# Top-k attention and two MLPs on one core: scores in native float32 by row halves, and other token pieces

## The reference

```python
# q, k, v: (4, 8, 576, 64); top_k = 32
scores = scale * np.matmul(q, k.transpose(0, 1, 3, 2))
kth = np.partition(scores, -top_k, axis=-1)[..., -top_k:-top_k + 1]
scores = np.where(scores >= kth, scores, -1000000000.0)
attn = np.exp(scores - np.max(scores, axis=-1, keepdims=True))
attn = attn / (np.sum(attn, axis=-1, keepdims=True) + 1e-09)
x = np.matmul(attn, v)                        # then (2304 tokens, 512)
gate = 1.0 / (1.0 + np.exp(-(x @ w_gate)))    # 512 -> 1536
y = gate * (x @ w_val) @ w_out                # -> 512
r = np.maximum(y @ w2_in, 0.0)                # -> 2048
out = (r * r) @ w2_out                        # -> 512
```

## Time and profile before

| | us |
|---|---|
| median of three runs | 1310.2 (1307.43 to 1312.79) |
| profiled execution | 1313.2 |
| its span | 1311.4 |

### The profile page before, as it was taken

How to read it: one execution, slowest core, us unless ns; L and a number is a source line. 1 busy time by engine, 2 the same in 40 slices (tenths; PEclk the granted TensorE clock), 3 DMA queues, 4 the chain that set the end, 5 groups by cost and what they waited for, 6 DMA issues and landing times.

```text
span 1311.4 us, 22472 instructions
## 1 busy us (share of the span) xinstructions
PE 1208.8 (92%) x7744; PEld 1083.6 (83%) x7744; DVE 842.9 (64%) x1692; ACT 807.9 (62%) x1806; POOL 654.1 (50%) x619
## 2 busy tenths in 40 slices
PE   3669888878998979999999999999999999999999
PEld 2558777878998879999989888887788888887999
DVE  6886796846767765787899567677863444640121
ACT  5986766757677766765786677657764443541221
POOL 6974557655655845552674455435634431430221
PEclk9779898989999989999999999999999999999999
DMA  5894665666666476655566554554455645556998
GB/s 187 315 311 132 213 223 197 217 237 230 233 228 212 169 261 240 216 191 190 176 215 214 205 181 155 187 181 157 155 182 200 208 167 174 172 174 197 344 364 302
DMA packets 89249, 279.08 MB, mean 213 GB/s; under 512 B 9904, under 2 KB 11952, under 8 KB 89136
## 3 DMA queue, kind: packets, MB, share of 16 engines
q1 hardware_dynamic: 89136, 277.65, 61.5%
HBM read 237.24 MB, written 40.37 MB: 212 GB/s over the span
## 4 chain that ended last, share of the span: by engine, by line
PE 69%; DMA 9%; POOL 8%; ACT 7%; issue 4%; DVE 2%; SPq 1%; ACTq 0%; POOLq 0%; DVEq 0%
PE ps L486 18%; PE ps L488 17%; PE ps L487 17%; PE ps L421 4%; PE ps L405 4%; PE ps L393 4%; DMA raw<-qk_in 4%; DMA ring<-w_in 3%; PE ps L472 3%; DMA w_split<-ring 2%; POOL ring L735 2%; POOL below L740 2%; POOL klo L721 1%; POOL qkh L726 1%; PE ps L415 1%
## 5 line engine op out<-in xcount | busy, mean ns | idle before, releaser
L740 POOL TENSOR_TENSOR below<-scores,below 128x576 f32<-128x576 f32 x144 | 207.3, 1440 | 247.1 <-ACT below L538 246.8
L659 DVE MAX8 top<-work 128x8 f32<-128x576 f32 x432 | 313.1, 753 | 4.9
L486 PE MATMUL ps<-xy_hi,ring 128*128 128x512 f32 (+3 forms) x800 | 290.0, 362 | 2.5 <-POOL xy_lo L764 1.7
L488 PE MATMUL ps<-xy_hi,ring 128*128 128x512 f32 (+3 forms) x800 | 282.9, 354 | 0.0
L487 PE MATMUL ps<-xy_lo,ring 128*128 128x512 f32 (+3 forms) x800 | 282.7, 353 | 0.0
L661 DVE MATCH_REPLACE8 work<-top,work 128x576 f32<-128x576 f32 x288 | 214.0, 743 | 0.0
L486 PE MATMUL ps<-g_hi,ring 128*128 128x512 f32 (+3 forms) x560 | 202.7, 362 | 2.9 <-POOL ring L735 2.8
L488 PE MATMUL ps<-g_hi,ring 128*128 128x512 f32 (+3 forms) x560 | 197.9, 353 | 0.0
L487 PE MATMUL ps<-g_lo,ring 128*128 128x512 f32 (+3 forms) x560 | 197.9, 353 | 0.0
L486 PEld LDWEIGHTS ps<-xy_hi,ring 128*128 128x128 f32 x800 | 151.0, 189 | 22.0 <-issue 6.2
L686 DVE SCALAR_TENSOR_TENSOR full_buf<-act_buf,ps 128x512 f32<-128x512 f32 (+3 forms) x60 | 35.6, 594 | 206.8 <-PE ps L488 201.8
(11 more groups left out here) (67 smaller groups left out, 2212.0 us busy)
## 6 DMA issues: line engine op xcount, KB each, us to landing
ring<-w_split SPq DMA_DIRECT2D x318, 512.0 KB, 3.8
w_split<-ring SPq DMA_DIRECT2D x68, 512.0 KB, 3.8
ring<-w_in SPq DMA_DIRECT2D x113, 256.0 KB, 3.5
vt<-v_in SPq DMA_DIRECT2D x32, 320.0 KB, 3.4
raw<-qk_in SPq DMA_DIRECT2D x16, 480.0 KB, 4.7
raw<-qk_in SPq DMA_DIRECT2D x16, 448.0 KB, 4.3
raw<-qk_in SPq DMA_DIRECT2D x8, 576.0 KB, 6.2
raw<-qk_in SPq DMA_DIRECT2D x8, 512.0 KB, 4.5
```

The lines of the kernel that those rows point to most:

```text
L486: nc.tensor.matmul(dst, w_hi, hi[:, k, 0:WIDTH[c]], start=first, stop=False)
L488: mm = nc.tensor.matmul(dst, w_lo, hi[:, k, 0:WIDTH[c]], start=False, stop=final)
L659: nc.vector.max(out=best, in_=sc if step == 0 else wk).then_inc(sel_step[t % 2], 1)
L740: nc.gpsimd.tensor_tensor(out=below[:, t % 2, :], in0=scores[:, t % 4, :], in1=below[:, t % 2, :], op=ALU.subtract).then_inc(mask_done, 1)
```

## The change

- The pieces become 128, 256, 384, 512, 512 and 512 tokens. There are still 144 tiles and 80 units with 16 halves; the MLPs start at slots 11, 28, 52, 84 and 116, and the last piece's 512 tokens come after attention. There are 36 groups instead of 32.
- Scores are native float32 matmuls straight from the loaded data. `heads_in` holds q twice (rows 0 to 63 and 64 to 127), the first half of the keys on rows 0 to 63 and the second on rows 64 to 127. A tile is two matmuls of 64 rows and 288 columns, one for each half of the rows, into different banks; a half tile is four, of 64 rows by 64 stationary columns.
- `split_head` goes from ScalarE and GpSimd, and so do `raw`, `qkh` and `klo`. A group's two heads are loaded two groups ahead, after the scores of the group that used the buffer.
- RING goes from 6 to 8 and AHEAD from 4 to 5; the first 23 splits begin at slot 0 instead of 2. GpSimd's `split_x` comes after the first evacuations of a slot.
- `pe_ns`, by which `shares()` deals out the MLP, is as before.

```diff
-CHUNK_BLOCKS = (3, 6, 7, 8, 8, 4)
+CHUNK_BLOCKS = (2, 4, 6, 8, 8, 8)
...
-RING = 6
-AHEAD = 4
+RING = 8
+AHEAD = 5
...
-for _g in range(1, NG):
-    for _h in range(2):
-        HEADS_AT.setdefault(max(FIRST_TILE[_g] - 5 + _h, FIRST_TILE[_g - 1] - 2, 0), []).append((_g, _h))
+for _g in range(2, NG):
+    HEADS_AT.setdefault(max(FIRST_TILE[_g - 1] - 2, 0), []).append(_g)
...
-    SPLIT_AT.setdefault(2 + _k // 2, []).append(_k)
+    SPLIT_AT.setdefault(_k // 2, []).append(_k)
...
+            def load_heads(g):
+                if g >= 2:
+                    sp.wait_ge(s_scored, FIRST_TILE[g - 1])
+                for h in range(2):
+                    sp.dma_start(heads_in[:, 2 * (g % 2) + h, 0:B64 * GROUPS[g][4] + HALF],
+                                 qk_of(g, h)).then_inc(heads_loaded[g % 2], 16)
...
             def score(t):
                 u, part = TILES[t]
                 g, i = UNITS[u][1], UNITS[u][3]
-                heads = [0, 1] if part == 2 else [part]
-                pe.wait_ge(qk_lo_done, 2 * g + heads[-1] + 1)
+                pe.wait_ge(heads_loaded[g % 2], 32 * (g // 2 + 1))
                 wait(pe, s_copied, t)
-                q = q_columns(g)
-                for half in range(2):
-                    dst = ps[:, half, 0:HALF]
-                    done, steps = 0, 2 * len(heads)
-                    for h in heads:
+                q = B64 * GROUPS[g][4]
+                for step in range(2 if part == 2 else 1):
+                    for half in range(2):
+                        rows = slice(DH * half, DH * half + DH)
+                        if part == 2:
+                            h = (half + step) % 2
+                            out_rows, n = slice(B64 * h, B64 * h + B64), B64
+                        else:
+                            h, out_rows, n = part, slice(0, P), P
                         r = 2 * (g % 2) + h
-                        at = P * i + (B64 if part == 2 and h == 0 else 0)
-                        for rhs in (qkh[:, r, q + half * HALF:q + (half + 1) * HALF],
-                                    klo[:, r, half * HALF:(half + 1) * HALF]):
-                            mm = nc.tensor.matmul(dst, qkh[:, r, at:at + P], rhs, start=(done == 0),
-                                                  stop=(done == steps - 1))
-                            done += 1
+                        mm = nc.tensor.matmul(ps[out_rows, half, 0:HALF], heads_in[rows, r, P * i:P * i + n],
+                                              heads_in[rows, r, q:q + HALF], start=True, stop=True)
                 mm.then_inc(s_scored, 1)
...
-                for g, h in HEADS_AT.get(s, []):
-                    split_head(g, h)
```

More of the change, by code:

```diff
@@ L58 @@
 CHUNK_END = [max(END[u] for u in range(NU) if UNITS[u][0] == c) for c in range(NC)]
[L61 to L70, removed]
+QMAX = max(B64 * GROUPS[g][4] for g in range(NG))
+QK_AT = [sum(2 * P * (B64 * GROUPS[h][4] + HALF) for h in range(g)) for g in range(NG + 1)]
 VCOLS = 2 * KFULL * DH + P
-QK_AT = [sum(2 * P * (q_columns(h) + SEQ) for h in range(g)) for g in range(NG + 1)]
 KT = 4
@@ L183, in sem @@
             return ctx.enter_context(nc.semaphore(name))
-        raw = sb("raw", [P, 2, QMAX + SEQ])
-        qkh = sb("qkh", [P, 4, QMAX + SEQ], F32R)
-        klo = sb("klo", [P, 4, SEQ], F32R)
+        heads_in = sb("heads_in", [P, 4, QMAX + HALF])
         vt = sb("vt", [P, 2, VCOLS])
@@ L232, in qk_of @@
         def qk_of(g, h):
-            cols = q_columns(g) + SEQ
+            cols = B64 * GROUPS[g][4] + HALF
             at = QK_AT[g] + h * P * cols
@@ L248, in attention_mlps @@
         const_ready = sem("const_ready")
-        raw_loaded = [sem("raw_loaded0"), sem("raw_loaded1")]
+        heads_loaded = [sem("heads_loaded0"), sem("heads_loaded1")]
         v_loaded = [sem("v_loaded0"), sem("v_loaded1")]
@@ L255, in attention_mlps @@
         w_lo_done = sem("w_lo_done")
-        qk_hi_done = sem("qk_hi_done")
-        k_lo_done = sem("k_lo_done")
-        qk_lo_done = sem("qk_lo_done")
         s_scored = sem("s_scored")
@@ L348, in mlp_dma @@
                                      act_buf[:, m % 2, 0:WIDTH[c]]).then_inc(out_stored[m % 2], 16)
-            load_head(0, 0)
-            load_head(0, 1)
+            load_heads(0)
+            load_heads(1)
             load_v(0)
@@ L358, in _ @@
                     mlp_dma(blocks_of(SHARES[s - 1][2]))
-                for g, h in (HEADS_AT.get(0, []) if s == 0 else []) + HEADS_AT.get(s + 1, []):
-                    load_head(g, h)
+                for g in HEADS_AT.get(s, []):
+                    load_heads(g)
                 if s in V_AT:
@@ L513, in _ @@
         def _(act):
[L514 to L521, removed]
             def copy_scores(t):
@@ L618, in _ @@
             nc.scalar.activation(rp[:, 0, 0:1], ident[:, 0:1], ACT.Exp)
-            split_head(0, 0)
-            split_head(0, 1)
             copy_scores(0)
@@ L716, in _ @@
         def _(pool):
[L717 to L729, removed]
             def split_weights(k):
@@ L803, in _ @@
                     normalise(UNIT_AT[s - NORM])
+                for c, n in blocks_of(SHARES[s - 1][2]) if s else []:
+                    evac(c, n)
                 for c, p in X_AT.get(s, []):
                     split_x(c, p)
[L806 to L809, removed]
                 for k in SPLIT_AT.get(s, []):
@@ L826 @@
     kt = k.reshape(heads, SEQ, DH).transpose(0, 2, 1)
-    qk_a = np.zeros(QK_AT[NG], np.float32)
+    qk_a = np.empty(QK_AT[NG], np.float32)
     for g, (c, b, p, at, n, col) in enumerate(GROUPS):
-        fc, qc = full_columns(g), q_columns(g)
-        part = qk_a[QK_AT[g]:QK_AT[g + 1]].reshape(2, 2, DH, qc + SEQ)
+        qc = B64 * n
+        part = qk_a[QK_AT[g]:QK_AT[g + 1]].reshape(2, 2, DH, qc + HALF)
         for h in range(2):
             hd = b * HEADS + 2 * p + h
-            part[h, :, :, :fc] = qt[hd, :, B64 * at:B64 * at + fc]
-            if n % 2:
-                part[h, :, :, fc + B64:fc + 2 * B64] = qt[hd, :, B64 * at + fc:B64 * (at + n)]
-            part[h, :, :, qc:] = np.roll(kt[hd], B64 * h, axis=1)
+            part[h, :, :, :qc] = qt[hd, :, B64 * at:B64 * at + qc]
+            part[h, :, :, qc:] = np.roll(kt[hd], B64 * h, axis=1).reshape(DH, 2, HALF).transpose(1, 0, 2)
     v_in = v.reshape(heads // 2, 2, SEQ, DH)
```

## The result

The changed kernel takes 1360.95 us (median of 4 runs, 1360.26 to 1364.21) where the kernel before takes 1311.49: the ratio is 1.038, with a 95% interval of 1.034 to 1.042. The forecast was 1288, with a range that ended at 1335. The profiled execution has a span of 1358.3 us.

A forecast was written before the change was run, and what follows sets the result against it. Bounds: the attention chain to 102.1 us, late split weights to 503.4, then TensorE. Start 71, small stages 302, then 212 + 264 + 250 + 190 made 1289 us of span, time 1288, range 1248 to 1335.

The forecast's parts named there:

- What bounds the kernel now: Whole kernel before: attention chain to 102.1 us, late split weights to 503.4, then TensorE, busy for all but 8.2 us.
- The start: Attention before the first MLP matmul: 71 us for 102.1, VectorE's 5.5 us a tile being late next.
- Two row halves at once: Full score tile: its two native matmuls on different rows overlap, 0.48 us of work instead of 0.97.
- The rival that they do not overlap: Score tiles: halves run one after the other, 0.48 us more a tile, 1342 us in all; chance 0.12.
- its milder form: Score tiles: halves overlap only in part, 0.24 us more a tile, 1315 us; no chance of its own.
- The switch of tiling: Score tiles: entering and leaving row tiling costs about 0.1 us each way, 0.19 a tile, 0.67 with the work.
- Half tiles: The 16 half tiles: 1.15 us each with quarters run in pairs (0.67 if four at once), for 1.06 before.
- SyncE's queue in the 128-token stage: Every third block costs 3.8 us of landing and 4 x 0.43 of issue; with 12 other DMAs 132 us.
- Rival B: Small stages: SyncE's queue and stores bind more; landings 1.5 us later add 36 us, 1325 in all; chance 0.16.
- The factor of 1.2 on TensorE's need: 128- and 256-token stages: TensorE's need of 252 us times the earlier stages' 1.2 gives 302, bounds 265 and 340.
- Ring of 8, splits 5 ahead: 256-token stage: loads asked for two block steps earlier, so ScalarE's 38.6 us of waiting falls under 10.
- The sum: Whole kernel: the stretches' forecasts add up to 1289 us of span for 1311.4, time 1288.

The follow-up runs named there:

- e1: The kernel before with only the new pieces and first splits from slot 0 (old scores, ring of 6, splits 4 ahead): span 1402 us, ratio 1.067.
- e4: The changed kernel with ring of 6 instead of 8 and splits 4 ahead instead of 5: span 1384 us, ratio 1.058.
- e7: The changed kernel with both key halves multiplied from rows 0 to 63: stretches 3 to 5 took 228.1, 288.0, 264.7 us for 213.0, 273.0, 252.5.
- e9: e5 with splits 3 blocks ahead instead of 5: median 1300.36 us, ratio 0.993 to the kernel before.
- e5: The changed kernel with the refill behind a store issued three block steps after it instead of one: span 1312 us, ratio 1.005 to the kernel before.
- e6: e5 with the old pieces 192, 384, 448, 512, 512, 256: median 1274.87 us, ratio 0.972 to the kernel before.

## Why the prediction was wrong, step by step

- *What bounds the kernel now:* right. TensorE after 503 us, the making of split weights in the small stages.
- *The start:* forecast 71, measured 64.3. The term "0.1 to 0.2 us a slot" for the splits of q and k was the wrong size: e1 and e4 have the same pieces and ring and differ in the scores, and start at 85.6 and 67.3, 18 us in 11 slots, of which the sum gave 3 at the start and 2 after it. ScalarE's copy of tile 11 started at 53.85 us instead of 64, and the slots took 4.4 us instead of 5.3: VectorE, which was to be late next, did not take the gain back. From there to the first MLP matmul it took 10.5 us instead of 7.6.
- *Two row halves at once:* right, shown by e7. The rival that they do not overlap was wrong, and so was its milder form: with 3 x 0.24 us of work instead of 0.48 and the 0.41 of switching, a tile would take 1.13 us, and it takes 0.89.
- *The switch of tiling:* mechanism right, size wrong. Forecast 0.19 a tile, measured 0.41. The earlier trace rows was read only up to the first MLP matmul after the products with v; the further 0.1 us lies between that matmul and the next, and another 0.1 between the two pairs of score records (in the trace's single records their starts are 0.35 apart, where 0.24 is the work). Over the 82 full tiles of stretches 3 to 5 this makes 18 us more than forecast, less 2 for the 8 half tiles, and the last four stretches took 928.5 for 916. Stage by stage the agreement is loose (213.0 for 212, 273.0 for 264, 252.5 for 250), so the near agreement of the totals is partly luck.
- *Half tiles:* forecast 1.15, measured 0.86.
- *SyncE's queue in the 128-token stage:* this is the step that failed. The cycle was there, with its floor of 132 us. But the landing of 3.8 us was the mean of a stage in which the queue at times rested ahead of a store, and without that rest each store lands behind loads just issued: 91.3 us in 20 waits is 4.6 each. (That loads just issued are what delays a store is read from the rests and landings of both kernels; no run changed the loads alone.) Loads at two other lines, which the sum had not counted, waited 18.4 us for stores: 12.1 of it in the refills of blocks split ahead of the first MLP, whose end now falls into the stage. So there are 110 us of standing instead of the 87 of the sum's 23 x 3.8; 110 issues at 0.43 are another 47, and 5 us are other waits. Rival B named this mechanism and gave it 0.16. It said +36 for landings 1.5 us later, and the small stages were 63.5 longer with waits only 0.8 us longer. By B's own sum that would be 45 x 0.8 less 31 us to spare, or +5: the spare time was not there.
- *The factor of 1.2 on TensorE's need:* wrong in kind. The traffic, the issues and the 23 splits of a stage do not shrink with its tokens. A piece of 128 tokens has the same of them as one of 192 and less matmul work to hide them, so the factor of the larger piece could not be carried over. This is the term that the forecast rested on: taken for each stage, 1.2 gives 109 us (91 x 1.2) for 128 tokens, less than the queue's floor of 132 in the same sum, and 193 for 256. Measured were 162.0 and 203.5, a factor of 365.5 / 252 = 1.45. TensorE alone was busy for 298.7 us in the two, not 252, at granted clocks of 0.85 and 0.92.
- *Ring of 8, splits 5 ahead:* ScalarE's wait was to fall under 10 us and was 36.0. The load was asked for two steps earlier only by the queue's own count, and the queue was late. e9 does what was forecast, with 1.4.
- *The sum:* e9, with the queue mended, has 123 + 183 = 306 us in the small stages for the 302 forecast, and 1297 for 1289. So the forecast is about right for this change with a queue that keeps up and splits 3 ahead. The parts agree less well: 123 and 183 us for 109 and 193, a start of 63 for 71, and 929 for 916 in the rest. The agreement of the sum is partly luck. Of the 63.5 us by which the small stages missed, the later refills took back 45 and the later split 14.
- *What of it is worth most:* not asked. The pieces and the scores should have been priced apart: the pieces cost 68 us and the rest gains 21.

## What to carry to other kernels

Work that is fixed for each piece (loads, splits, stores, their issue in one queue) can set a lower bound for a stage; before a piece is made smaller, add up that fixed work and compare it with what the smaller piece leaves to hide it. A queue in program order should not be made to wait for a store that it has just issued: moving the dependent load two block steps back, into the slack of the ring, was worth 46 us of span with the new pieces (e5) and 17 with the old ones (e6), without moving a byte less. The cost of a new kind of instruction in a stream is read from the last old one before it to the second old one after it, for part of it can lie behind the first.

## What was not expected of the hardware

- Two float32 matmuls of 64 rows that run at once in a stream of full-array matmuls cost 0.89 us and the same two over all 128 rows, one after the other, 0.97: 0.41 us of changing the tiling used up nearly all of the overlap's 0.48.
- Four matmuls of 64 rows by 64 columns run at once, in 0.86 us with the changes of tiling, no more than two of 64 by 128.
- A 512 KB store that was issued after a rest of the queue let its refill go after 2.3 us, and after 4.2 to 5.0 where three loads had just been issued ahead of it; over the whole kernel its median landing, on the page of the profile, went from 3.8 to 4.7 us with the change.
- In the 128-token stage TensorE's granted clock was 0.85 of full speed, in the same stage of e5 0.91 and of e9 0.95. Waiting for loads costs twice: after 2.71 us of it the granted clock was 0.50 and nine transposes took 1.92 us instead of 0.90. Of the 38 us that the later refills took out of the stage, 14 were busy time of TensorE with the same matmuls.
